# A Fourier filter and two dense layers in one kernel: filters kept on chip, another order of first loads, other banks and a split last tile

## The reference

```python
X = np.fft.rfft(x, axis=1)               # x: (2, 3008, 256)
y = np.fft.irfft(X * (filt_r + 1j * filt_i), n=3008, axis=1)
x = y.reshape(6016, 256)
h = x @ moe_w_in                         # 256 -> 2048
x = np.where(h > 0, h, exp(min(h, 0)) - 1) @ moe_w_out      # 2048 -> 256
h = x @ moe2_w_in
out = (h * clip(h + 3, 0, 6) / 6) @ moe2_w_out
```

## Time and profile before

| what | us |
|---|---|
| median of 3 runs | 1119.72 (1117.58 to 1120.87) |
| the profiled execution's own time | 1119.74 |
| span in the profile | 1117.9 |
| busy: PE, ACT, DVE, POOL | 1106.2, 750.9, 743.9, 289.9 |

### The profile page before, as it was taken

The page is one execution under the profiler, slowest core; times in us unless marked ns, Lnnn a source line. Parts: engine busy times, 40 slices in busy tenths (PEclk is TensorE's granted clock), DMA queues, the critical chain, the costliest instruction groups (busy, mean ns, idle before and its releaser), DMA issues.

```text
span 1117.9 us, 13357 instructions
## 1 busy us (share of the span) xinstructions
PE 1106.2 (99%) x4840; PEld 891.0 (80%) x4840; DVE 743.9 (67%) x912; ACT 750.9 (67%) x1113; POOL 289.9 (26%) x228
## 2 busy tenths in 40 slices
PE   8999999999999999999999999999999999999998
PEld 4666788888888888888888788888888888888886
DVE  6777466666667666666677866666666665666665
ACT  0222588888788888888899766665666566666654
POOL 3877402102102111111288821111120120120000
PEclk9999999999999999999999999999999999999999
DMA  9977300200200200200311200200101001100000
GB/s 251 278 254 240 114 1 1 74 1 1 74 1 0 74 1 1 74 1 1 112 38 57 93 1 1 74 1 25 50 1 37 37 1 37 38 1 1 38 1 37
DMA packets 31185, 59.30 MB, mean 53 GB/s; under 512 B 3600, under 2 KB 19856, under 8 KB 31120
## 3 DMA queue, kind: packets, MB, share of 16 engines
q1 hardware_dynamic: 24784, 48.10, 13.2%
q10 hardware_dynamic: 6336, 10.36, 2.7%
HBM read 39.94 MB, written 18.51 MB: 52 GB/s over the span
## 4 chain that ended last, share of the span: by engine, by line
PE 91%; ACT 4%; DVE 2%; issue 1%; DMA 1%; POOL 0%; ACTq 0%
PE ps L390 43%; PE ps L381 13%; PE ps L380 13%; PE ps L379 13%; PE ps L347 2%; PE ps L322 2%; PE ps L338 2%; PE ps L339 2%; PE ps L330 2%; DVE e L643 1%; ACT e L516 1%; DMA w_raw<-w_dev 1%; ACT e L518 1%; ACT w_hi L495 1%; DVE g_lo L657 1%
## 5 line engine op out<-in xcount | busy, mean ns | idle before, releaser
L657 DVE TENSOR_TENSOR g_lo<-e,g_hi 128x502 fp32r<-128x502 f32 (+1 forms) x288 | 277.9, 992 | 136.0 <-ACT g_hi L548 135.8
L381 PE MATMUL ps<-op_lo,w_hi 128*128 128x502 f32 x672 | 261.9, 390 | 0.0
L379 PE MATMUL ps<-op_hi,w_hi 128*128 128x502 f32 x672 | 261.8, 390 | 0.0
L380 PE MATMUL ps<-op_hi,w_lo 128*128 128x502 f32 x672 | 261.2, 389 | 0.0
L390 PE MATMUL ps<-g_hi,w_hi 128*128 128x502 f32 x768 | 236.3, 389 | 2.0 <-ACT ystage L487 2.0
L390 PE MATMUL ps<-g_lo,w_hi 128*128 128x502 f32 x768 | 237.3, 390 | 0.9 <-DVE g_lo L657 0.7
L390 PE MATMUL ps<-g_hi,w_lo 128*128 128x502 f32 x768 | 235.5, 387 | 0.0
L726 POOL TENSOR_TENSOR op_lo<-op_raw,op_hi 128x1004 fp32r<-128x1004 f32 (+1 forms) x48 | 100.4, 2091 | 490.5 <-ACT op_hi L503 490.5
L390 PEld LDWEIGHTS ps<-g_hi,w_hi 128*128 128x128 f32 x768 | 144.0, 188 | 31.8 <-ACT ystage L487 2.4
L390 PEld LDWEIGHTS ps<-g_lo,w_hi 128*128 128x128 f32 x768 | 143.7, 188 | 31.8 <-DVE g_lo L657 3.2
L390 PEld LDWEIGHTS ps<-g_hi,w_lo 128*128 128x128 f32 x768 | 144.5, 188 | 29.3
(11 more groups left out here) (53 smaller groups left out, 1149.6 us busy)
## 6 DMA issues: line engine op xcount, KB each, us to landing
f_ring<-f_dev SPq DMA_DIRECT2D x32, 384.0 KB, 4.6
op_raw<-y SPq DMA_DIRECT2D x36, 251.0 KB, 3.6
x_ring<-x_dev SPq DMA_DIRECT2D x32, 192.0 KB, 5.1
y<-ystage SPq DMA_DIRECT2D x12, 502.0 KB, 2.8
out_dev<-ystage SPq DMA_DIRECT2D x12, 502.0 KB, 2.8
y<-ystage ACTq DMA_DIRECT2D x24, 235.0 KB, 3.1
w_raw<-w_dev ACTq DMA_DIRECT2D x16, 256.0 KB, 4.7
w_raw<-w_dev SPq DMA_DIRECT2D x16, 256.0 KB, 3.0
```

What stands on the lines that cost most here:

```text
L379: pe.matmul(out, w_hi[p][:, cols], hi, start=start, stop=False, skip_group_check=True)
L380: pe.matmul(out, w_lo[p][:, cols], hi, start=False, stop=False, skip_group_check=True)
L381: pe.matmul(out, w_hi[p][:, cols], lo, start=False, stop=True, skip_group_check=True).then_inc(done, 1)
L657: return dve.tensor_tensor(g_lo[:, tiles, :], e[:, tiles, :], f32(g_hi[:, tiles, :]), ALU.subtract)
```

## The change

- **Filters.** The eight filters of the first chunk get a place of their own (`f_kept`) and serve the third chunk again. The last chunk runs its groups in reverse order, so its first three groups find their filters still in the ring. 21 filters are loaded and get signs, not 32. `f_kept` overlaps the operand buffers of dense block 0, so `load_xr(0)` also waits until the third chunk's products are done, and it and the operand's preparation are placed one step earlier.
- **First loads.** `sign` and the filters 0 and 1 are issued by ACT. SP issues A, x0, BX, x1, the other matrices, x2, x3, f2, x4, f3, x5, f4, x6, f5, x7, f6, f7 with no waits between them. There are two warm-up matmuls, not three.
- **Banks.** The pieces of the last chunk go to banks 2 and 3, not 0 and 1; the first down product no longer waits for all of them to be copied out, the second does.
- **Last tile.** The last down product finishes output half 0 before half 1 and ACT copies and SP stores each half by itself.

```diff
-FIRST_OP = NG - NOP - 1
+FIRST_OP = NG - NOP - 2
+def group_of(i):
+    c, g = ORDER[i // GROUPS], i % GROUPS
+    return c, (GROUPS - 1 - g if i // GROUPS == len(ORDER) - 1 else g)
+KEEP_END = GROUPS
+RING_END = 2 * GROUPS
+REUSE_END = 3 * GROUPS + FSLOTS
+def filter_loaded_at(i):
+    if i < RING_END:
+        return i
+    if i < 3 * GROUPS:
+        return i - 2 * GROUPS
+    if i < REUSE_END:
+        return RING_END - 1 - (i - 3 * GROUPS)
+    return i
...
+            f_kept = sbuf(early, "f_kept", [P, GROUPS, 2, XCOL])
...
         def ps_i(n):
-            return ps[:, n % 2, 0:IJ * ICOL]
+            return ps[:, 2 + (n - LAST_I) % 2 if n >= LAST_I else n % 2, 0:IJ * ICOL]
...
             def load_f(i):
-                if i >= FSLOTS:
-                    sp.wait_ge(prod_ready, i - FSLOTS + 1)
-                sp.dma_start(f_ring[:, i % FSLOTS].rearrange("p a n -> p (a n)"),
-                             f_dev[c // B, :, g]).then_inc(f_loaded[i % FSLOTS], 16)
+                dst = filt(i).rearrange("p a n -> p (a n)")
+                if i < KEEP_END:
+                    sp.dma_start(dst, f_dev[c // B, :, g]).then_inc(f_kept_loaded[i], 16)
+                elif filter_loaded_at(i) == i:
+                    if i >= KEEP_END + FSLOTS:
+                        sp.wait_ge(prod_ready, i - FSLOTS + 1)
+                    sp.dma_start(dst, f_dev[c // B, :, g]).then_inc(f_loaded[ring_slot(i)], 16)
...
             load_x(1)
-            sp.dma_start(sign[:], sign_dev).then_inc(sign_loaded, 16)
+            sp.dma_start(mats[:, 2 * P:], mats_dev[:, 2 * P:]).then_inc(mat_loaded["back"], 16)
             load_x(2)
-            load_f(0)
-            sp.dma_start(mats[:, 2 * P:], mats_dev[:, 2 * P:]).then_inc(mat_loaded["back"], 16)
             load_x(3)
-            load_f(1)
+            load_f(2)
             load_x(4)
-            load_f(2)
-            for i in range(5, XSLOTS):
-                load_x(i)
+            load_f(3)
+            load_x(5)
+            load_f(4)
+            load_x(6)
+            load_f(5)
+            load_x(7)
+            load_f(6)
+            load_f(7)
...
             for i in range(NG):
-                if FSLOTS <= i + FSLOTS - 1 < NG:
+                if KEEP_END <= i + FSLOTS - 1 < NG:
                     load_f(i + FSLOTS - 1)
...
                 if i == FIRST_OP - 2:
+                    sp.wait_ge(prod_ready, 3 * GROUPS)
                     load_xr(0)
...
-            store_out(2 * NS - 1, 1)
+            at = (NS - 1) * 2 * T + T
+            for o in range(DH):
+                sp.wait_ge(end_evac[o], 1)
+                sp.dma_start(out_dev[o, :, at:at + T], ystage[:, 1, o * T:o * T + T]).then_inc(y_stored[1], 16)
...
-            for _ in range(3):
+            for _ in range(2):
                 pe.matmul(ps[:, 0, :], back[:, 0, 0, :], back[:, 0, 0:4, :].rearrange("p j d -> p (j d)"),
...
                 pe.wait_ge(hi_ready, v + 1)
+                if v == NU - 1 and done is d12_done:
+                    pe.wait_ge(lo_ready, v + 1)
+                    for o in range(DH):
...
+                        last.then_inc(last_half if o == 0 else d12_done, 1)
+                    return
...
                 if v == 0:
-                    pe.wait_ge(i_evac, NPIECE)
+                    pe.wait_ge(i_evac, LAST_I)
...
+                if v == 0:
+                    pe.wait_ge(i_evac, NPIECE)
                 if v >= 0:
                     if v and v % PAIRS == 0:
                         pe.wait_ge(out_evac[1], v // PAIRS)
...
+            def evacuate_last():
+                wait_stage_stored(act, 2 * NS - 1, 1)
+                act.wait_ge(last_half, 1)
+                act.activation(ystage[:, 1, 0:T], out_bank(0, 1), ACT.Copy, scale=1.0 / 6.0).then_inc(end_evac[0], 1)
+                act.wait_ge(d12_done, NU)
+                act.activation(ystage[:, 1, T:2 * T], out_bank(1, 1), ACT.Copy, scale=1.0 / 6.0).then_inc(end_evac[1], 1)
...
+            act.dma_start(sign[:], sign_dev).then_inc(sign_loaded, 16)
+            for i in range(2):
+                c, g = group_of(i)
+                act.dma_start(f_kept[:, i].rearrange("p a n -> p (a n)"),
+                              f_dev[c // B, :, g]).then_inc(f_kept_loaded[i], 16)
...
-                if i + 2 < NG:
+                if i + 2 < NG and filter_loaded_at(i + 2) == i + 2:
                     apply_sign(i + 2)
```

More of the change, by code:

```diff
@@ L53, with ring_slot @@
 NOP = len(OP_PIECES)
-FIRST_OP = NG - NOP - 1
+FIRST_OP = NG - NOP - 2
[13 more added lines that the diff above has]
+    return i
+def ring_slot(i):
+    if i < RING_END:
+        return (i - KEEP_END) % FSLOTS
+    return (RING_END - 1 - (i - 3 * GROUPS) % FSLOTS - KEEP_END) % FSLOTS
 def crt(k1, k2):
@@ L110, in build @@
         w_raw = sbuf(ctx, "w_raw", [P, 2, 12 * P])
+        with ExitStack() as early:
+            f_kept = sbuf(early, "f_kept", [P, GROUPS, 2, XCOL])
         op_hi = [sbuf(ctx, "op0_hi", [P, 7, T], F32R)]
@@ L167, in build @@
         x_loaded = [sem(f"x_loaded{k}") for k in range(XSLOTS)]
+        f_kept_loaded = [sem(f"f_kept_loaded{k}") for k in range(GROUPS)]
         f_loaded = [sem(f"f_loaded{k}") for k in range(FSLOTS)]
@@ L190, in build, with filt, ring_loads, wait_filter @@
         lo11, lo12, lopair = sem("lo11"), sem("lo12"), sem("lopair")
+        last_half = sem("last_half")
+        end_evac = [sem("end_evac0"), sem("end_evac1")]
         out_evac = [sem("out_evac0"), sem("out_evac1")]
         y_stored = [sem("y_stored0"), sem("y_stored1")]
-        def group_of(i):
-            return ORDER[i // GROUPS], i % GROUPS
+        def filt(i):
+            if filter_loaded_at(i) < KEEP_END:
+                return f_kept[:, i % GROUPS]
+            return f_ring[:, ring_slot(i)]
+        def ring_loads(i):
+            return sum(1 for k in range(KEEP_END, filter_loaded_at(i) + 1)
+                       if filter_loaded_at(k) == k and ring_slot(k) == ring_slot(i))
+        def wait_filter(eng, i):
+            if filter_loaded_at(i) < KEEP_END:
+                eng.wait_ge(f_kept_loaded[i % GROUPS], 16)
+            else:
+                eng.wait_ge(f_loaded[ring_slot(i)], 16 * ring_loads(i))
+        def signs_done(i):
+            return sum(1 for k in range(filter_loaded_at(i) + 1) if filter_loaded_at(k) == k)
         def piece_at(i):
@@ L311, in _ @@
             store_out(2 * NS - 1, 0)
-            store_out(2 * NS - 1, 1)
+            at = (NS - 1) * 2 * T + T
+            for o in range(DH):
+                sp.wait_ge(end_evac[o], 1)
+                sp.dma_start(out_dev[o, :, at:at + T], ystage[:, 1, o * T:o * T + T]).then_inc(y_stored[1], 16)
             sp.wait_ge(y_stored[0], 16 * 2 * NS)
-            sp.wait_ge(y_stored[1], 16 * 2 * NS)
+            sp.wait_ge(y_stored[1], 16 * (2 * NS + 1))
         @block.tensor
@@ L343, in part_i @@
                 pe.wait_ge(back_ready, GROUPS * (pos + 1))
-                if n >= 2:
+                if LAST_I <= n < LAST_I + 2:
+                    pe.wait_ge(spec_ready, NG)
+                elif n >= 2:
                     pe.wait_ge(i_evac, n - 1)
@@ L394, in down @@
                 pe.wait_ge(hi_ready, v + 1)
+                if v == NU - 1 and done is d12_done:
+                    pe.wait_ge(lo_ready, v + 1)
+                    for o in range(DH):
+                        at = (7 + 2 * fi + o) * P
+                        cols = slice(at, at + P)
+                        pe.matmul(out_bank(o, t), w_hi[p][:, cols], g_hi[:, tile, :], start=False, stop=False,
+                                  skip_group_check=True)
+                        pe.matmul(out_bank(o, t), w_lo[p][:, cols], g_hi[:, tile, :], start=False, stop=False,
+                                  skip_group_check=True)
+                        last = pe.matmul(out_bank(o, t), w_hi[p][:, cols], g_lo[:, tile, :], start=False, stop=True,
+                                         skip_group_check=True)
+                        last.then_inc(last_half if o == 0 else d12_done, 1)
+                    return
                 add(w_hi, g_hi, start and p == 0, False)
@@ L597, in _ @@
                 if p == 0 and u:
-                    evacuate(s - 1)
+                    if u < NU:
+                        evacuate(s - 1)
+                    else:
+                        evacuate_last()
         @block.vector
@@ L611, in products @@
                     dve.wait_ge(r_done, i - 1)
[L612 to L615, removed]
+                wait_filter(dve, i)
+                dve.tensor_tensor(prod_r[:, i % 2, :], ps_x(i), filt(i)[:, 0, :], ALU.mult)
+                dve.wait_ge(signed, signs_done(i))
+                dve.tensor_tensor(prod_i[:, i % 2, :], ps_x(i), filt(i)[:, 1, :],
                                   ALU.mult).then_inc(prod_ready, 1)
@@ L622, in turn_r @@
                     dve.wait_ge(i_done, PIECES * (pos - 1))
+                g = group_of(i)[1]
```

(4 more changed lines are left out.)

## The result

The changed kernel takes 1121.03 us (median of 20 runs, 1119.87 to 1123.89); the kernel before, on the same chip, 1119.63 (20 runs, 1117.58 to 1123.03). The ratio is 1.0015, 95% interval 1.0008 to 1.0021: slower by about 1.4 us where the forecast was +6.9. The profiled execution took 1121.14 us, its span is 1119.0 (before 1119.74 and 1117.9).

A forecast was written before the change was run, and what follows sets the result against it. PE, busy 1106.2 of 1117.9 us, was taken as the bound, with the early stall hanging on weight block 0's landing. On 1119.74: +5.5 + 2.0 - 0.5 - 0.1 = +6.9, so 1126.6 us; range 1118.0 to 1129.0.

The forecast's parts named there:

- a line in order of issue: First loads: both DMA queues act as one line, the last comer waiting for all bytes ahead; given 0.60.
- the 5.5 us: First loads: product 4 starts later by 5.5 us, bounds +4.2 and +6.4, as weight block 0 lands late.
- The landing: Weight block 0's second load, behind SP's filters and x: lands at 25.0 to 27.2 us, before at 20.8.
- the 2.8 us that I added behind the 4.24 MB: First loads: delay from the last weight byte moved to its landing, read from the kernel before.
- The rival with the short line: First loads: only about 1.1 MB can stand ahead, block 0 again takes 9.9 us; 1119.9 us, chance 0.17.
- Its +0.8 at product 4: Short-line case: product 4 is late by as much as product 0, about 0.8 us.
- The rival with queues that share: First loads: engines serve both queues in turn, weights land by 18 to 19; 1118.5 us, chance 0.20.
- The start: First matmuls: x1 lands at 8.1 to 9.4, first R about 1.4 us late, the removed warm-up gains nothing.
- Low clock behind product 4, +2.0: PE idles 4 to 7 us before product 4, restarts at half speed: +2.0 us, bounds 0 and 2.7.
- The dense start, -0.5: Where dense layers begin: PE's wait moves to ACT's copy of P1, P6 earlier by 0.5 us, bounds 0 and -0.5.
- Late filters and operand, 0: Filter 27, sign(28) and load_xr(0) come late or wait without cost: 0, bounds 0 and 1.
- The end, -0.1: Last stores: DMA engines are full, so the shorter second copy is hidden: -0.1 us, bounds 0 and -0.5.

The follow-up runs named there:

- a_warm5: The changed kernel with five warm-up matmuls in place of two: 1125.34 us (7 runs), ratio 1.0039 to the kernel before.
- a_f1_sp_warm3: The changed kernel with filter 1 issued by SP behind x2 instead of by ACT, and three warm-up matmuls: 1123.41 us, ratio 1.0034 to the kernel before.
- b_banks: The kernel before with only the new banks and waits for the last pieces: 1118.74 us, ratio 0.9993.
- b_last: The kernel before with only the last tile split by halves: 1120.03 us, ratio 1.0001.

## Why the forecast was wrong

**The failed step is the first loads: "a line in order of issue", and the 5.5 us that came from it.** The landing was put at 25.0 to 27.2; it was 21.75 (13.35 + 8.4). The row that I leaned on, SP's 0.01 MB from 33 to 34, was a true observation of a backlog below 1.3 MB, and I carried it to one of 2 MB and more. The trace of the kernel before spoke against one line too, and I had not counted it. These are its queues from 0 to 20.85 us, when the second weight load landed:

```profile
q1 hardware_dynamic: 2770, 4.53, 79.4%
q10 hardware_dynamic: 288, 0.52, 9.4%
```

SP had issued 3.69 MB by 10.92 (the 3.10, filter 3 and x8). It moved 4.53, so 0.8 MB that it issued later went ahead of the landing. That, and not a delay behind the last byte, fills much of the 2.8 us that I added behind the 4.24 MB.

The rival with the short line had the mechanism, and I gave it 0.17. Worked with 1.35 MB it comes out, though this figure is taken from the same traces: issue at 3.28 MB moved, first byte at 4.6 MB, about 17.5 us, then 0.52 MB at half of some 0.3 MB a us, 3.5 us: 21.0 for the last byte, landed at 21.75. Its +0.8 at product 4 met the measured 0.90 by luck: it had the load issued 0.8 us later and as long under way as before, and it was issued 2.43 later and took 1.5 less. The rival with queues that share was right only behind the common part. There the Trainium skill's rule of turns between queue rows (DMA: Bandwidth & Descriptors, "Queues, rings and completion order") agrees with the trace: 0.19 MB each from 19 to 20. It does not hold for the 4 us before.

**The start.** x1 was put at 8.1 to 9.4 and landed at 8.5: right. The first R was put 1.4 us late and came 3.6 late: this term of the sum was mis-sized. 0.91 is A(1)'s later begin (8.54 against 7.63). The other 2.69 are A(1), X(0), A(2) and X(1) at half speed: between their starts lie 1.87, 1.28, 1.70 and 0.97 us, before 0.90, 0.72, 0.86 and 0.65. I counted the removed warm-up as free because PE waits for x1 anyway. It wasn't: with five warm-ups (a_warm5) PE was busy from 1.45 us without a gap and ran the four records of A(0) and A(1) in 1.72 us, at full speed; with two, and the gaps for x, full speed came only near 13.4. The granted clock reads 1.00 in this stretch, so it has to be read from the records' lengths. I also hid this shift inside the 5.5; without the weight load it is the chain itself.

**Low clock behind product 4, +2.0.** Didn't occur, as the gap did not. That such a gap can cost this is shown by a_warm5: after its wait of 2.9 us, R ran 1.65 and 1.28 for 0.65 twice, 1.6 us in the two alone. That it needn't is shown by a_f1_sp_warm3, where 3.0 us of waiting left the clock at 1.00.

**What the late start gave back.** Products 0 to 3 became late by as much as product 4 used to be, so PE's two waits (2.0) went. I had this as a gain only in the rival. And a later pace keeps SP from issuing one x and one filter ahead of block 1. The two kernels that mend the start without touching block 1 are the slower ones: 1.0039 and 1.0034. With block 1 issued early it is 0.9981.

**The dense start, -0.5.** Right: -0.48 by P6, with the wait on the copy of P1 that was named; b_banks 0.9993 agrees and can't be told from none.

**Late filters and operand, 0.** Right for this kernel: no wait of PE between 40 and 117 us. Sign(28) is late as I said, DVE waits 0.75 us for it at 109.16, and PE doesn't.

**The end, -0.1.** Not told from none: the first of the last stores is issued 1.03 later and the span is 1.1 longer, b_last is 1.0001. From the end of the last matmul to the end of the span it is 5.4 us, and 5.6 in b_last, for 5.3 before.

With the landing right, the terms of the forecast and of its rival give 1.4 - 2.0 - 0.5 - 0.1 = -1.2, that rival's 1118.5. The start, put at 1.4 and measured at 3.6, makes that +1.0, against 1.1 in the profiled pair and 1.4 in the medians. So two terms failed: the landing, which gave too much, and the start, which gave too little. That the result still lies inside the stated range comes of the range's width, not of the sum.

## What to carry to other kernels

A row that shows one line in order shows it up to the backlog of that row; before carrying it to a deeper one, count how much stood ahead and price the case that it ends there. Warm-up work in front of a wait is not free because the engine waits anyway: ask at which speed the work behind the wait runs. And when a late start is mended, look for the next transfer in line: here the mend was worth nothing until the second weight block was issued early.

## What the runs showed of the hardware

Two engines' DMA queues went in the order of issue for the first 1.30 to 1.38 MB that stood ahead (seven kernels), or for all of it when it was 0.6 to 1.0 MB (four; a filter issued in the same 0.01 us not counted), and shared from there (0.24 and 0.17 MB, then 0.19 each, in two stretches of 1 us). DMAs of half the size (1.37 MB) or rows of half the size (1.30) made little difference. The granted-clock column showed 1.00 over the first 13 us while matmul records took 0.85 to 1.04 us per 512 columns (2.08 and 1.71 for two) where they took 0.43 later. After a wait of 2.9 us the granted clock was 0.50 (a_warm5), after one of 3.0 it stayed at 1.00 (a_f1_sp_warm3).
